# The last head's weighted sum in two halves, GpSimd's last two splits back to back, and fewer unread products in the first ranking, in a fused attention, routing and two-layer kernel

## The reference

```python
mask = q_bucket[:, :, :, None] == k_bucket[:, :, None, :]
scores = np.where(mask, scale * np.matmul(q, k.transpose(0, 1, 3, 2)), -1000000000.0)
attn = np.exp(scores - np.max(scores, axis=-1, keepdims=True))
attn = attn / (np.sum(attn, axis=-1, keepdims=True) + 1e-09)
x = np.matmul(attn, v)                      # then (tokens, heads * 64)
...
order = np.argsort(-(x @ w_gate).flatten())
for idx in order:                           # greedy, cap = N // E per expert
    tok, e = (int(idx) // E, int(idx) % E)
    if assigned[tok] >= 0 or counts[e] >= cap:
        continue
    assigned[tok] = e
    counts[e] += 1
...
out[mask] = np.maximum(x[mask] @ w1[e], 0.0) @ w2[e]
...
h = x @ w_in
return (h * (1.0 / (1.0 + np.exp(-h)))) @ w_out
```

## Time and profile before

| | |
|---|---|
| time, median of 3 executions | 775.11 us (773.96 to 776.61) |
| the profiled execution | 777.72 us, its span 775.9 us |
| PE busy | 744.7 us, 96% of the span |
| DVE, ACT, POOL busy | 481.1, 268.1, 156.4 us |
| mean granted clock of PE | 0.99 of full speed |

### The profile page before, as it was taken

The page is one execution under the profiler, slowest core; times in us unless marked ns, Lnnn a source line. Parts: engine busy times, 40 slices in busy tenths (PEclk is TensorE's granted clock), DMA queues, the critical chain, the costliest instruction groups (busy, mean ns, idle before and its releaser), DMA issues.

```text
span 775.9 us, 19348 instructions
## 1 busy us (share of the span) xinstructions
PE 744.7 (96%) x7778; PEld 629.4 (81%) x7785; DVE 481.1 (62%) x1097; ACT 268.1 (35%) x551; POOL 156.4 (20%) x193
## 2 busy tenths in 40 slices
PE   8799999999998899999999999999999999999996
PEld 4577777777777569999999999978887888878885
DVE  4788888888889888797797740653233323242321
ACT  4768767767765012222222212221013101211111
POOL 5443545545643011010010000000002000010001
PEclk9899999999999899999999999999999999999999
DMA  7265565565533063463463477500001000010001
GB/s 151 46 121 119 123 139 118 122 139 126 114 106 86 22 236 112 137 219 136 137 206 149 136 247 277 183 0 1 1 1 54 0 0 0 0 54 0 0 0 54
DMA packets 58194, 75.07 MB, mean 97 GB/s; under 512 B 28736, under 2 KB 43072, under 8 KB 57120
## 3 DMA queue, kind: packets, MB, share of 16 engines
q1 hardware_dynamic: 54592, 67.12, 30.3%
q0 software_dynamic: 2208, 7.21, 2.9%
q10 hardware_dynamic: 1344, 0.04, 0.1%
HBM read 64.92 MB, written 6.29 MB: 92 GB/s over the span
## 4 chain that ended last, share of the span: by engine, by line
PE 86%; issue 4%; DVE 3%; DMA 2%; ACT 2%; POOL 1%; DVEq 0%; SPq 0%; ACTq 0%; POOLq 0%
PE quad_ps L1527 17%; PE quad_ps L1416 10%; PE quad_ps L1428 10%; PE quad_ps L1249 9%; PE score_ps L1510 8%; PE quad_ps L1510 8%; PE score_ps L1234 5%; PE score_ps L1235 4%; PE work_ps L1358 3%; PE work_ps L1220 2%; PE quad_ps L1258 2%; DMA area<-x_rows,ids_now 1%; DMA experts_w<-in_k 1%; PE pv_ps L1202 1%; DVE area L1030 1%
## 5 line engine op out<-in xcount | busy, mean ns | idle before, releaser
L1527 PE MATMUL quad_ps<-y_s,w_in_s 128*128 128x512 f32 x576 | 137.8, 390 | 2.7 <-DVE y_s L1152 2.0
L1527 PEld LDWEIGHTS quad_ps<-y_s,w_in_s 128*128 128x128 f32 x576 | 107.9, 188 | 26.2 <-DVE y_s L1152 2.8
L1170 DVE TENSOR_TENSOR gate<-quad_ps,sig 128x512 f32<-128x512 f32 x48 | 33.2, 692 | 145.9 <-ACT sig L656 145.9
L870 DVE TENSOR_SCALAR_CACHE_REDUCE att_area<-score_ps 128x768 f32<-128x768 f32 x96 | 91.9, 957 | 39.1 <-PE score_ps L1235 37.4
L524 ACT ACTIVATE att_area<-att_area 128x768 f32<-128x768 f32 x96 | 90.1, 939 | 46.0 <-DVE att_area L870 44.8
L656 ACT ACTIVATE sig<-quad_ps 128x512 f32<-128x512 f32 x48 | 28.7, 598 | 210.5 <-PE quad_ps L1527 210.5
L1416 PE MATMUL quad_ps<-area,experts_w 128*128 128x192 f32 x512 | 96.1, 334 | 1.5 <-ACT area L616 1.2
L1428 PE MATMUL quad_ps<-area,experts_w 128*128 128x192 f32 x512 | 87.2, 328 | 0.0
L1416 PEld LDWEIGHTS quad_ps<-area,experts_w 128*128 128x128 f32 x512 | 81.8, 190 | 2.1 <-ACT area L616 2.1
L1428 PEld LDWEIGHTS quad_ps<-area,experts_w 128*128 128x128 f32 x512 | 82.9, 190 | 0.0
L1234 PE MATMUL score_ps<-k_parts,q_parts 128*128 128x512 f32 x192 | 72.9, 380 | 10.3 <-DVE att_area L870 10.0
(11 more groups left out here) (204 smaller groups left out, 1104.6 us busy)
## 6 DMA issues: line engine op xcount, KB each, us to landing
experts_w<-in_moe_w SPq DMA_DIRECT2D x16, 2048.0 KB, 9.5
att_area<-in_v SPq DMA_DIRECT2D x64, 192.0 KB, 3.8
experts_w<-in_moe_w_in SPq DMA_DIRECT2D x8, 512.0 KB, 5.4
w_out_raw<-in_moe_w_out SPq DMA_DIRECT2D x4, 1024.0 KB, 8.3
experts_w<-in_k SPq DMA_DIRECT2D x16, 192.0 KB, 3.3
experts_w<-in_q SPq DMA_DIRECT2D x16, 192.0 KB, 3.6
k_bits<-k_parts SPq DMA_DIRECT2D x16, 192.0 KB, 4.6
x_rows<-att_area SPq DMA_DIRECT2D x8, 384.0 KB, 3.1
```

What stands on the lines that cost most here:

```text
L870: nc.vector.tensor_scalar(probs[c % 3], score_ps[0][:, 0:S], 0.5 * BIG, None, ALU.min, ALU.min, accum_out=neg_max[:, c:c + 1]).then_inc(s_ ...
L1170: nc.vector.tensor_tensor(gate[:, :], layer_ps[f % 2][:, 0:GT], sig[:, :], ALU.mult).then_inc(s_mul, 1)
L1527: done = nc.tensor.matmul(layer_ps[f % 2][:, 0:GT], w_in_s[:, a, w_cols], y_s[:, c, b, :], start=(c == 0 and a + b == 0), stop=(c == DC - ...
```

## The change

Five edits. On PE, in the last pair with p = 1, head 14's sum is dealt out as `LAST_SHARE = [8, 8, 0, 8, 0, 0]`. Head 15's sum is made in two halves, tiles 0 to 2 and tiles 3 to 5: each goes through all 24 blocks and 4 quarters, with 96 columns in place of 192; the first stands at the end of the pair, behind `x_rows` of head 14, the second behind the pair. ACT's copy of head 14's sum comes ahead of both copies of the row; its copy of head 15's sum is in two halves, ahead of the scaling of head 14's rows (L588), and `x_rows` of head 15 takes three tiles behind each half. On POOL both last splits stand ahead of `add_logits`. In the first ranking the unread products behind i = 8, 9, 10 are 3, 2, 0 in place of 4, 4, 4: seven fewer.

```diff
-            def turned(h):
+            def turned(h, ts=slice(0, T)):
...
-                        if t == T - 1 and not (first and p == 0):
+                        if t == (T - 2 if last and p == 1 else T - 1) and not (first and p == 0):
...
-                        if last and p == 1 and t >= T - 2:
-                            first_batch_row_out(t - (T - 2))
+                        if last and p == 1 and t == T - 2:
+                            first_batch_row_out(0)
+                            first_batch_row_out(1)
...
             act.wait_ge(s_x_full, HEADS - 1)
+            for half in range(2):
+                turned(HEADS - 1, slice(half * (T // 2), (half + 1) * (T // 2)))
...
             x_half.then_inc(s_x_free, 1)
-            turned(HEADS - 1)
...
                     if last and p == 1:
-                        split_beside(PAIRS - 2, h)
+                        for i in (PAIRS - 2, PAIRS - 1):
+                            split_beside(i, h)
                     if not first:
                         add_logits(h - 2)
-                    if last and p == 1:
-                        split_beside(PAIRS - 1, h)
...
-                pe.wait_ge(s_turned, h + 1)
-                for t in range(T):
+                pe.wait_ge(s_turned, h + 1 + (ts[0] > 0))
+                for t in ts:
...
-            def weighted(h, p, b0, n, loads):
+            def weighted(h, p, b0, n, loads, t0=0, t1=T):
...
-                    pe.wait_ge(s_pt, T * h + T)
+                    pe.wait_ge(s_pt, T * h + t1)
...
-                        done = nc.tensor.matmul(quad_ps[side, 512 * a:512 * a + QT],
+                        done = nc.tensor.matmul(quad_ps[side, 512 * a + Q * t0:512 * a + Q * t1],
...
-                                                probs_t[p][rows, :, Q * b:Q * (b + 1)], start=(b < 2), stop=(b >= KB - 2))
-                if n and b0 + n == KB:
+                                                probs_t[p][rows, t0:t1, Q * b:Q * (b + 1)], start=(b < 2), stop=(b >= KB - 2))
+                if n and b0 + n == KB and t1 == T:
...
             SHARE = [4, 4, 0, 12, 4, 0]
+            LAST_SHARE = [8, 8, 0, 8, 0, 0]
...
+                        if last and p == 1 and t == T - 1:
+                            pe.wait_ge(s_row, 2)
+                            x_rows(HEADS - 2, work_banks[0])
+                            weighted(HEADS - 1, 1, 0, KB, PAIRS - 1, 0, T // 2)
...
-            pe.wait_ge(s_row, 2)
-            x_rows(HEADS - 2, work_banks[0])
-            weighted(HEADS - 1, 1, 0, KB, PAIRS - 1)
-            x_rows(HEADS - 1, work_banks[1])
+            weighted(HEADS - 1, 1, 0, KB, PAIRS - 1, T // 2, T)
+            for half in range(2):
+                x_rows(HEADS - 1, work_banks[1], None, range(half * (T // 2), (half + 1) * (T // 2)))
...
-                keep_busy(4 if T - 1 <= i < NT - 1 else 0, layer_ps[0])
+                keep_busy({5: 4, 6: 4, 7: 4, 8: 3, 9: 2}.get(i, 0), layer_ps[0])
```

More of the change, by code:

```diff
@@ L526, in exp_tile @@
                                      accum_out=row_sum[:, c:c + 1]).then_inc(s_exp, 1)
-            def turned(h):
+            def turned(h, ts=slice(0, T)):
                 act.wait_ge(s_pv, h + 1)
-                nc.scalar.activation(weighted_t.rearrange("p (t a j) -> p a t j", t=T, j=Q), sums_ps, ACT.Copy).then_inc(s_turned, 1)
+                dst = weighted_t.rearrange("p (t a j) -> p a t j", t=T, j=Q)
+                nc.scalar.activation(dst[:, :, ts, :], sums_ps[:, :, ts, :], ACT.Copy).then_inc(s_turned, 1)
             for i in range(4):
@@ L1211, in fill_work, with x_rows @@
                 last.then_inc(s_work_full, 1)
-            def x_rows(h, bank, free=None):
+            def x_rows(h, bank, free=None, ts=range(T)):
                 rhs = to_x[:, h % H, :] if isinstance(h, int) else to_x[:, bass.ds(h % H, 1), :].rearrange("p a e -> p (a e)")
@@ L1217, in x_rows @@
                     pe.wait_ge(s_work_free, free)
-                pe.wait_ge(s_turned, h + 1)
-                for t in range(T):
+                pe.wait_ge(s_turned, h + 1 + (ts[0] > 0))
+                for t in ts:
                     last = nc.tensor.matmul(bank[:, t * DE:(t + 1) * DE], weighted_t[:, t * P:(t + 1) * P], rhs, start=True, stop=True)
-                last.then_inc(s_x_full, 1)
+                if ts[-1] == T - 1:
+                    last.then_inc(s_x_full, 1)
             def scores(c, h, n, crossed):
@@ L1311, in pair, with weighted_part @@
                         if len(ev[t]) < 2:
-                            weighted_part(h, p, t, first, g)
+                            weighted_part(h, p, t, first, g, LAST_SHARE if last and p == 1 else SHARE)
+                        if last and p == 1 and t == T - 1:
+                            pe.wait_ge(s_row, 2)
+                            x_rows(HEADS - 2, work_banks[0])
+                            weighted(HEADS - 1, 1, 0, KB, PAIRS - 1, 0, T // 2)
                         if last and (p == 0 and t >= T - 2 or p == 1 and t < 2):
                             keep_busy(2, work_banks[1])
-            def weighted_part(h, p, t, first, g):
+            def weighted_part(h, p, t, first, g, share=SHARE):
                 if not (first and p == 0):
-                    weighted(h - 1, 1 - p, sum(SHARE[0:t]), SHARE[t], g if p else g - 1)
+                    weighted(h - 1, 1 - p, sum(share[0:t]), share[t], g if p else g - 1)
             pair(0, True, False)
```

## The result

| | before | changed |
|---|---|---|
| median of 12 executions each, same chip | 775.65 us (773.96 to 778.32) | 779.65 us (777.21 to 782.49) |
| the profiled execution | 777.72 us, span 775.9 | 779.02 us, span 777.3 |

The ratio of the changed kernel to the one before is 1.0052, with a 95% interval of 1.0040 to 1.0065: **4.0 us slower** (3.1 to 5.0). The forecast was +0.6, with a range up to 777.8 us, so it was wrong. So I compare single stretches of them, and whole times only by medians.

What follows compares the result with a forecast made beforehand. PE, busy 96% of the span, and a slackless chain of waits to head 15's rows were taken as the bound. 0 + 2.1 - 0.3 = +1.8, with -1.2 gave +0.6: 775.7 us, range 773.4 to 777.8.

Steps and rivals of the forecast that it cites:

- Part 2: Head 15's sum in two halves, 6.3 us at 17 ns a pair: +2.1 us, bounds 0 and +4.2.
- Rival C: Head 15's halves: a narrow record costs what a record costs now, +4.2 us, total 777.8 us; chance 0.14.
- Rival A: Head 15's sum: time goes with columns, the halves cost nothing, total 773.6 us; chance 0.22.
- Rival D: Head 15's sum: a floor of 25 ns per record, 9.6 us, total 779.0 us; chance 0.04.
- E: PE's clock: with thinner work the low level comes elsewhere or once more, some 2 us either way; chance 0.07.
- Part 1: Head 14's sum dealt earlier: last scores 1.3 us later, its `x_rows` unmoved; 0, bounds -0.1 and +0.4 us.
- Part 3: ACT's copy of head 15's sum in halves: `x_rows` starts 0.32 us earlier; -0.32, bounds -0.4 and 0.
- Part 4: POOL's last splits ahead of `add_logits`: DVE wins about 0.4 us but has 0.90 us of idle; worth 0.
- Part 5: Seven unread products fewer in the first ranking: -1.2 us for the median (0 to -1.9), -1.5 in the profiled execution.

Runs made afterwards that it cites:

- e6_copy_halves: The kernel before with only ACT's copy and `x_rows` of head 15 in halves behind the whole sum; 775.74 us, ratio 1.0003.
- e5_boundary_moved: The changed kernel with 32 unread products of 8 columns (64 instructions with loads) ahead of `x_rows` of head 14; 783.88 us, one execution only.
- e8_sum_twice: The kernel before with head 15's sum made twice over at the full 192 columns; 779.49 us over four executions, ratio 1.0051.
- e1_whole_sum: The changed kernel with head 15's sum in one piece again, copy and `x_rows` still in halves; 775.29 us, ratio 0.999.

## Why the prediction was wrong, by its own steps

**Part 2, the step that failed.** Its term was +2.1 us, 6.3 for the sum; the sum took 7.8, a term of +3.6, and outside the 5 to 7 us that the prediction gave itself. I had read from the weight loads that a pair of instructions comes every 17 ns, evenly, and took that for the limit. The runs show neither. In a group the pairs are 12.8 ns apart, faster than the 17. Behind it the supply comes in lots of 256 instructions, 3.45 to 3.84 us apart, so 27 to 30 ns a pair when it is drawn on for long. The earlier trace rows are sixteen loads from the middle of a sum that never idled, and the eight that are 17 ns apart come ahead of the eight that are 7 ns apart; the prediction had taken the quicker ones for the first, those that stood ready. Such steps inside a lot could say nothing on how often a lot comes. The 7.8 us are 2.05 + 1.86 + 1.66 of work, 2.23 of idle time. The upper bound of the term, +4.2, did hold it.

Rival C's price (+4.2) came near, for another reason: it supposed that a narrow record costs what a wide one costs, and it costs 12.8 ns. Rival A is nearly right within a lot (12.8 ns, where half of 20.3 is 10.2) and wrong over the sum. Rival D, a floor of 25 ns a record, is refuted by 128 records in 1.86 us. The same holds for the rule of the Trainium skill named in the prediction ("TensorE: Matmul & The Clock Gate", "Wait — 56ns, not 53.3ns?"): for records in a quarter of the array the trace disagrees, 12.8 ns on average at 96 columns and 20.3 at 192. (They start in groups of eight that overlap, so whether the rule holds for two matmuls in the same part of the array is not shown.) E did not happen: the ranking of the changed profile has one stretch at the low clock, of 6.8 us as before, and it lies later with the rest.

**Part 1** was forecast at 0, with a bound of +0.4. It was +0.65 in the profile, and +1.1 alone in the time (interval -0.2 to 2.4). The path behind the last scores was read rightly: from DVE's taking them to `x_rows` of head 14 it is 245.85 - 242.31 = 3.54 us, where the forecast had 245.6 - 241.88 = 3.72. What failed is how late the scores come, 2.15 us and not 1.3. The break behind 58 records of the second dealt part makes up the difference: from the start of the first dealt part to the next scores it is 235.62 - 233.88 = 1.74 us, from the start of the second 239.19 - 236.59 = 2.60, 0.86 more for the same work. Of these 0.86 the timeline shows 0.33 as idle, because it counts from the end of a record. It is the same cause again. How long the idle time is (0.33, 0.85, 1.11, 1.13 us in four kernels) goes with when the packet passes; what sets that stays open.

**Part 3** was forecast at -0.3. The mechanism is as told (two copies, DVE's wait 0.32 shorter in `e6_copy_halves`), its value below what the runs tell.

**Part 4**, forecast at 0: right. L882, the old L880, takes 0.13 us, and POOL's order alone gives a ratio of 1.0. What would have hidden it, DVE's idle time ahead of head 15's rows, was 4.68 us in the changed kernel.

**Part 5**, forecast at -1.2 for the median and -1.5 in the profiled execution: right, -1.3 alone, and 1.51 less between head 15's rows and the ranking's end. The 1.93 us of idle in the earlier trace rows were a backlog of unread products, and the supposition that executions with less of the low clock have less of it is borne out: 1.93, about 1.0 and 0.16 us of idle at 6.8, 3.4 and 0 us of it.

**The sum.** By the parts measured alone: +1.1 (part 1) + 3.4 (halves, copy included) + 0 (POOL) - 1.3 = +3.2 us, within the interval of 3.1 to 5.0. That is four medians, each with about 1.5 us to either side, and 0.46 of the +1.1 is not in the changed kernel, so the remaining 0.8 is no finding. In the profiled pair the ranking ends 2.04 us later (2.46 with the offset) while the times differ by 1.3. What lies between these two is less than the 4 to 5 us by which executions of one kernel differ.

What is shown: the place at which PE idles goes with a count of 256 instructions (`e5_boundary_moved`), whatever the columns (`e8_sum_twice`), and taking the instructions away takes the loss away (`e1_whole_sum`). What is argued only: that the idle time is the wait for a packet of the instruction queue. The sizes fit, and so do the distances at all twelve new starts, but no run changed how that queue delivers.

## What to carry to other kernels

Cutting matmuls in two narrower ones doubles their number, and a long run of short instructions can cost more than its columns. Here 256 instructions, loads included, that hold less than 3.4 to 3.8 us of work were too few for PE not to idle once the run was some hundreds of instructions long; 192 records in a row passed unseen. Count instructions per microsecond over a few hundred of them, not over sixteen, and look in the chain for "issue" inside one loop. Where an idle time of DVE ends with counting on PE, look for unread products ahead of it, and for what the clock was while they ran: that was the one part that paid, and it paid by how long the clock was low.

## What the runs showed of the hardware

PE got its instructions in lots of 256: with 384 records in a row it idled at records 144 and 272 of the sum, with 32 more instruction pairs ahead of it at 112, 240 and 368, and new lots began every 3.45 to 3.84 us (about 3.4 in `e8_sum_twice`). Twelve new starts in six kernels came 2.2 to 2.8 us behind a 16 KB packet of the instruction queue. A kernel can run this way unseen. The sum before, 192 records of 192 columns in 4.17 us, never idled, and the same kernel with two such sums idled 0.53 us at record 272.

Matmuls of 96 columns in quarters of the array (32 by 64) start 12.8 ns apart on average; of 192 columns 20.3 ns. So in a quarter the time of a record does go with its columns, though not fully by half.

Twenty-four unread products of 512 columns ahead of the ranking's end held up DVE by 1.93 us with 6.8 us at the low clock, by about 1.0 us with 3.4, and by 0.16 us with none.
